# Preparing the hidden layers' weights in the first batch of a fused attention, Fourier and feed-forward kernel

## The reference

```python
q_d, k_d, v_d = means of q, k, v over groups of 4 tokens          # 144 rows
out_up    = repeat(softmax(q_d @ k_d.T / 8) @ v_d, 4)
out_local = softmax(band |i - j| < 4 of q @ k.T / 8) @ v
x  = heads side by side of (out_up + out_local)                   # 576 x 512
u  = x + real(fft over tokens, then over columns)
un = (u - mean(u)) / sqrt(var(u) + 1e-6)
y  = u + relu(un @ w_ch1) @ w_ch2                                 # 512 x 2048, 2048 x 512
gate = sigmoid(causal 5-tap convolution of y, per column)
out  = (gate * (y @ w_val)) @ w_out
```

## Time and profile before

| what | us |
|---|---|
| three timed runs | 818.84, 819.88, 823.23 |
| their median | 819.88 |
| the profiled execution, whole | 816.47 |
| its span, first to last instruction | 814.7 |
| first matmul of the hidden layers starts | 140.17 |

### The profile page before, as it was taken

The page is one execution under the profiler, slowest core; times in us unless marked ns, Lnnn a source line. Parts: engine busy times, 40 slices in busy tenths (PEclk is TensorE's granted clock), DMA queues, the critical chain, the costliest instruction groups (busy, mean ns, idle before and its releaser), DMA issues.

```text
span 814.7 us, 15570 instructions
## 1 busy us (share of the span) xinstructions
PE 728.4 (89%) x5956; PEld 542.8 (67%) x5956; DVE 436.8 (54%) x955; ACT 204.7 (25%) x409; POOL 65.3 (8%) x82
## 2 busy tenths in 40 slices
PE   1838546799999998999999998999999999999998
PEld 1624225577776776787776776777776777777776
DVE  6838769744453585644553584643643681113552
ACT  1206585222221122222221122222211122111101
POOL 3000213000110210000100210000100210000000
PEclk9999555999999999999999999999999999999999
DMA  9991031702200103602200204513100000000001
GB/s 285 285 254 46 2 130 54 170 9 71 62 1 1 59 30 105 127 12 75 48 1 1 59 30 131 104 29 79 26 2 1 0 30 30 2 1 1 1 15 45
DMA packets 42106, 49.15 MB, mean 60 GB/s; under 512 B 4784, under 2 KB 35568, under 8 KB 40944
## 3 DMA queue, kind: packets, MB, share of 16 engines
q1 hardware_dynamic: 33392, 31.69, 16.1%
q10 hardware_dynamic: 8640, 16.43, 6.2%
HBM read 43.38 MB, written 4.72 MB: 59 GB/s over the span
## 4 chain that ended last, share of the span: by engine, by line
PE 72%; DVE 11%; DMA 6%; issue 6%; ACT 3%; POOL 1%; SPq 1%; ACTq 0%; DVEq 0%; POOLq 0%
PE P L499 21%; PE Y L515 21%; PE P L622 4%; PE Y L611 4%; PE Y L622 3%; PE A L524 3%; DMA kl<-qk_win 2%; PE A L486 2%; DMA shared<-v_pool 2%; PE A L479 2%; PE A L469 2%; PE A L411 1%; PE A L572 1%; PE A L422 1%; PE A L566 1%
## 5 line engine op out<-in xcount | busy, mean ns | idle before, releaser
L499 PE MATMUL P<-unT,w 128*128 128x288 f16 x1536 | 210.0, 287 | 8.7 <-issue 4.8
L515 PE MATMUL Y<-hT,w 128*128 128x288 f16 x1536 | 214.9, 286 | 1.5 <-DVE xT L1068 1.5
L1047 DVE SCALAR_TENSOR_TENSOR hT<-P,hT 128x288 f16<-128x288 f32 x128 | 58.3, 456 | 259.1 <-ACT hT L728 259.1
L499 PEld LDWEIGHTS P<-unT,w 128*128 128x128 f16 x1536 | 148.4, 98 | 52.4 <-issue 12.2
L515 PEld LDWEIGHTS Y<-hT,w 128*128 128x128 f16 x1536 | 144.8, 98 | 45.6 <-issue 7.0
L728 ACT ACTIVATE hT<-P 128x288 f16<-128x288 f32 x128 | 52.5, 410 | 193.5 <-PE P L499 193.4
L1083 DVE SCALAR_TENSOR_TENSOR gate<-xT,cw,gate 128x288 f32<-128x288 f32 x128 | 66.4, 519 | 4.5
L699 ACT ACTIVATE prob_or_un<-prob_or_un 73x288 f32<-73x288 f32 (+1 forms) x52 | 23.3, 449 | 141.4 <-DVE prob_or_un L918 141.4
L524 PE MATMUL A<-sdft,pair_or_folded 128*128 128x289 f32 (+5 forms) x102 | 32.7, 443 | 8.7 <-DVE pair_or_folded L975 8.7
L622 PE MATMUL P<-shared,wo 128*128 128x288 f32 x128 | 32.1, 409 | 0.7 <-DVE shared L1095 0.5
L622 PE MATMUL Y<-shared,wo 128*128 128x288 f32 x128 | 32.1, 409 | 0.5 <-DVE shared L1095 0.5
(11 more groups left out here) (147 smaller groups left out, 831.4 us busy)
## 6 DMA issues: line engine op xcount, KB each, us to landing
w<-w_ch ACTq DMA_DIRECT2D x8, 1024.0 KB, 12.0
kl<-qk_win SPq DMA_DIRECT2D x40, 140.0 KB, 5.2
ql<-qk_win SPq DMA_DIRECT2D x20, 256.0 KB, 4.9
vl<-v_win SPq DMA_DIRECT2D x72, 65.0 KB
pair_or_folded<-qk_pool SPq DMA_DIRECT2D x8, 580.0 KB, 4.9
pair_or_spectrum<-qk_pool SPq DMA_DIRECT2D x8, 580.0 KB, 5.3
out<-ot ACTq DMA_DIRECT2D x32, 144.0 KB, 1.8
x<-v_pool SPq DMA_DIRECT2D x4, 576.0 KB
```

Of the source, the lines that this page charges most:

```text
L499: last = mm(P[s % 2][:, 0:HN], w1s[:, k, f * 128:(f + 1) * 128, wt], unT[:, ut, k, ha * HN:(ha + 1) * HN], start=k == 0 and wt + ut == 0, ...
L515: last = mm(Y[d][:, 0:HN], w2s[:, f, d * 128:(d + 1) * 128, wt], hT[s % 3][:, ht, :], start=f == 0 and wt + ht == 0, stop=f == KF - 1 and ...
L1047: nc.vector.scalar_tensor_tensor(out=hT[s % 3][:, 1, :], in0=P[s % 2][:, 0:HN], scalar=0.0, in1=hT[s % 3][:, 0, :], op0=ALU.max, op1=ALU.s ...
```

## The change

- *Scales.* In place of the greatest magnitude, the sum of squares of the whole matrix sets the power of two. ScalarE squares each chunk into a scratch tile and accumulates the row sums (`weight_square`), in its slots 4 to 15 and around the spectrum copies. PE adds them over partitions with a matmul of ones (`weight_sum`), and DVE makes the scale in five operations. The exponents 5 and 13 become 10 and 14.
- *w1.* It is loaded two chunk places further on in a wider tile, so that a chunk's two halves, now side by side, go two places ahead and need no temporary and no copy. ScalarE makes the high halves. DVE makes the low halves of chunks 0, 2, 4, 6 in one operation each; GpSimd those of 1, 3, 5, 7 in two operations (scale, subtract), one before the folds and one after each of them. w_val is loaded into the last two places once w1 is split.
- *w2.* GpSimd alone splits it, after the last 1/sqrt, in four operations a chunk. The down matmuls now wait by chunk: hidden tile 0 for one chunk, tile 2 for two, tile 4 for four, tile 8 for all eight.
- *Values.* In the first batch GpSimd sums the value tiles in two additions each. Before that it does one very early tensor_tensor on a constant. The loop steps keep DVE's reduce.
- *Keys.* The third window of the first batch has its own buffers for queries and keys, in the tile that held the second value tile; GpSimd clears the key buffer once the values are summed. On SP's queue the value windows 3 and 4 come before the key windows 4 and 5. The identity has its own semaphore and is loaded earlier.
- *Weight loads.* w1 in ScalarE's slots 1 to 4; w2 in 7, 8, 13 and 14, and the transform tables in 13.

```diff
-HID_BITS, W2_BITS = 5, 13
+HID_BITS, W2_BITS = 10, 14
...
-POOLING_FIRST = {1: [("qk", 1)], 2: [("v", 0)], 3: [("v", 1), ("qk", 2)], 5: [("qk", 3)]}
-WEIGHT_LOADS = [2, 3, 4, 5, 6, 7, 9, 10, 8]
+POOLING_FIRST = {1: [("qk", 1)], 3: [("qk", 2)], 5: [("qk", 3)]}
+WEIGHT_LOADS = {1: [0], 2: [1], 3: [2], 4: [3], 7: [4], 8: [5], 13: [8, 6], 14: [7]}
+SQUARES = {4: 0, 5: 1, 6: 2, 7: 3, 8: 4, 9: 5, 10: 6, 11: 7, 12: 8, 13: 9, 14: 10, 15: 11}
+W1_HIGH = {12: [0, 1], 13: [2], 14: [3], 15: [4], 16: [5]}
+W1_LOW = {13: 0, 14: 2, 15: 4}
+W2_NEEDED = {0: 1, 2: 2, 4: 4, 8: 8}
 SEQ_AT, FEAT_AT = 24, 29
-W1_AT = 11
+W1_AT = 12
...
+def keys(b, t):
+    if opening(b) and t == 2:
+        return ql_first, kl_first, ld_qk_first, 1
+    i = (0, 1, 0, 0, 1)[t] if opening(b) else t % 2
+    if opening(b):
+        return ql[i][:], kl[i][:], ld_qk[i], (1, 1, 1, 2, 2)[t]
+    return ql[i][:], kl[i][:], ld_qk[i], b * (3 - i) + t // 2 + i
...
 def wchunk(c, part=None):
-    w, ws = ((w1, w1s), (w2, w2s))[c // WCH]
     if part is None:
-        return w[:].rearrange("p k f -> p (k f)")[:, c % WCH * WCW:(c % WCH + 1) * WCW]
-    return ws.rearrange("p k f t -> p (k f) t")[:, c % WCH * WCW:(c % WCH + 1) * WCW, part]
+        return w1_wv[:, c + 2, :] if c < WCH else w2c[:, c - WCH, :]
+    return (w1h if c < WCH else w2h)[:, c % WCH, (1 - part) * WCW:(2 - part) * WCW]
...
+        if opening(b):
             window(b, 2, "v")
-        window(b, 2, "qk")
-        window(b, 3, "qk")
-        if not later(b):
             window(b, 3, "v")
+            window(b, 3, "qk")
             window(b, 4, "qk")
             window(b, 4, "v")
         else:
+            window(b, 3, "qk")
             window(b, 2, "v")
...
-        if what == "v" and opening(b):
-            done = UD + 1 if t == 4 else 0
+        if opening(b):
+            done = (UD + 1 if t == 4 else 0) if what == "v" else (0, 0, 0, UD + 1, UD + 2)[t]
...
         if what == "qk":
-            sp.dma_start(ql[i][:], qk_win[b, t, :, :, 0:128]).then_inc(ld_qk[i], 16)
+            q_tile, k_tile, landed, _ = keys(b, t)
+            if opening(b) and t == 2:
+                sp.wait_ge(zeroed, 7)
+                sp.sem_inc(passed, 1)
+            sp.dma_start(q_tile, qk_win[b, t, :, :, 0:128]).then_inc(landed, 16)
             for j in range(2):
-                sp.dma_start(kl[i][D * j:D * j + D, :, j, :], qk_win[b, t, D * j:D * j + D, :, 128:128 + 2 * WK]).then_inc(ld_qk[i], 16)
+                sp.dma_start(k_tile[D * j:D * j + D, :, j, :], qk_win[b, t, D * j:D * j + D, :, 128:128 + 2 * WK]).then_inc(landed, 16)
         else:
             tile, landed, _ = values(b, t)
...
+            if s in W2_NEEDED:
+                pe.wait_ge(w2_split, W2_NEEDED[s])
             if s == 0:
-                pe.wait_ge(w_split, 2 * WCH)
                 pe.wait_ge(step_over, b + 1)
...
+    def weight_sum(i):
+        pe.wait_ge(w_squares, WCH * (i + 1))
+        mm((A[0], P[0])[i][:, 0:WCH], one.to_broadcast([128, 128]), wsum[:, i, :], start=True, stop=True).then_inc(w_all, 1)
...
+                if s == W1_AT:
+                    weight_sum(0)
...
                 mix_feat(b, j)
+                if j == 0:
+                    weight_sum(1)
...
+            w, dram = ((wv, w_val), (wo[:], w_out))[c - 2 * KD - 1]
+            if c == 2 * KD + 1:
+                for done in w1_split:
+                    act.wait_ge(done, WCH // 2)
+            act.dma_start(w, dram.rearrange("(k p) f -> p k f", p=128)).then_inc(ld_wvo, 16)
...
     def weight_high(c):
-        i = c // WCH
-        if c % WCH == 0:
-            act.wait_ge(w_scale, i + 1)
-        nc.scalar.activation(wtmp[:, c % 2, :], wchunk(c), ACT.Copy, scale=wscale[:, i:i + 1]).then_inc(w_high, 1)
-    def weight_in_place(c):
-        act.wait_ge(w_low, c + 1)
-        nc.scalar.copy(wchunk(c, 0), wtmp[:, c % 2, :]).then_inc(w_split, 1)
-    def weights(c):
+        if c == 0:
+            act.wait_ge(w_scale, 1)
         if c >= 2:
-            weight_in_place(c - 2)
-        if c < 2 * WCH:
-            if c >= 2:
-                act.wait_ge(w_split, c - 1)
-            weight_high(c)
+            act.wait_ge(w1_split[c % 2], c // 2)
+        nc.scalar.activation(wchunk(c, 0), wchunk(c), ACT.Copy, scale=wscale[:, 0:1]).then_inc(w_high, 1)
+    def weight_square(c):
+        if c % 2 == 0:
+            act.wait_ge(ld_w[c // 2], 16)
+        if c > 0:
+            act.wait_ge(w_squares, c)
+        nc.scalar.activation(gate[:].rearrange("p d c -> p (d c)")[:, 0:WCW], wchunk(c), ACT.Square,
+                             accum_out=wsum[:, c // WCH, c % WCH:c % WCH + 1]).then_inc(w_squares, 1)
     def gate_e(b, ha):
         act.wait_ge(tap_done, 8 * TAPS * b + 4 * TAPS * (ha + 1))
...
             if m is None:
-                if s in WEIGHT_LOADS:
-                    load_weights(WEIGHT_LOADS.index(s))
+                for c in WEIGHT_LOADS.get(s, []):
+                    load_weights(c)
...
-            if m is None and W1_AT <= s < W1_AT + WCH:
-                weights(s - W1_AT)
+            if m is None:
+                for c in W1_HIGH.get(s, []):
+                    weight_high(c)
+                if s in SQUARES:
+                    weight_square(SQUARES[s])
...
                 gate_e(m, 0)
         if m is None:
-            for c in range(S0 + NU + LAG_AV - W1_AT, WCH):
-                weights(c)
-            load_weights(2 * KD + 1)
-            load_weights(2 * KD + 2)
-            for c in range(WCH, WCH + 4):
-                weights(c)
+            for c in range(WCH + 4, WCH + 6):
+                weight_square(c)
             for g in range(5):
                 spectrum(b, g)
+            for c in range(WCH + 6, 2 * WCH):
+                weight_square(c)
+            for c in range(6, WCH):
+                weight_high(c)
+            load_weights(2 * KD + 2)
             for j in range(3):
-                weights(WCH + 4 + j)
                 odd_part(b, j)
+            load_weights(2 * KD + 1)
             for i in range(6):
                 u_columns(b, i, m)
-                if i == 1:
-                    weights(WCH + 7)
                 un_columns(b, i)
-            for c in range(WCH + 8, 2 * WCH + 2):
-                weights(c)
...
     def weight_scale(i):
         dve.wait_ge(w_all, i + 1)
-        t = wtop[:, 1, i:i + 1]
+        t = wtop[:, i:i + 1]
         sc = wscale[:, i:i + 1]
+        nc.vector.tensor_reduce(t, (A[0], P[0])[i][:, 0:WCH], axis=AX.X, op=ALU.add).then_inc(w_chain, 1)
+        dve.wait_ge(w_chain, 5 * i + 1)
         nc.vector.tensor_scalar(t, t, 2.0 ** -100, None, ALU.max).then_inc(w_chain, 1)
-        dve.wait_ge(w_chain, 3 * i + 1)
-        nc.vector.tensor_scalar(t.bitcast(u32), t.bitcast(u32), 0x7F800000, None, ALU.bitwise_and).then_inc(w_chain, 1)
-        dve.wait_ge(w_chain, 3 * i + 2)
+        dve.wait_ge(w_chain, 5 * i + 2)
+        nc.vector.tensor_scalar(t.bitcast(u32), t.bitcast(u32), 1, 0x7F800000, ALU.logical_shift_right,
+                                ALU.bitwise_and).then_inc(w_chain, 1)
+        dve.wait_ge(w_chain, 5 * i + 3)
         nc.vector.reciprocal(sc, t).then_inc(w_chain, 1)
-        if i == 1:
-            nc.vector.tensor_scalar(unscale[:], wtop[:, 1, 0:1], t, 2.0 ** -(HID_BITS + W2_BITS), ALU.mult, ALU.mult)
-        dve.wait_ge(w_chain, 3 * i + 3)
-        nc.vector.tensor_scalar(sc, sc, 2.0 ** (HID_BITS, W2_BITS)[i], None, ALU.mult).then_inc(w_scale, 1)
+        dve.wait_ge(w_chain, 5 * i + 4)
+        nc.vector.tensor_scalar(sc, sc, 2.0 ** ((HID_BITS, W2_BITS)[i] - 64), None, ALU.mult).then_inc(w_scale, 1)
+        if i == 0:
+            dve.sem_inc(w_chain, 1)
+        else:
+            dve.wait_ge(w_scale, 2)
...
-        i = c // WCH
-        nc.vector.scalar_tensor_tensor(out=wchunk(c, 1), in0=wchunk(c), scalar=wscale[:, i:i + 1],
-                                       in1=wtmp[:, c % 2, :], op0=ALU.mult, op1=ALU.subtract).then_inc(w_low, 1)
+        nc.vector.scalar_tensor_tensor(out=wchunk(c, 1), in0=wchunk(c), scalar=wscale[:, 0:1], in1=wchunk(c, 0),
+                                       op0=ALU.mult, op1=ALU.subtract).then_inc(w1_split[0], 1)
     def hidden_low(b, s):
...
             if m is None:
-                if W1_AT - 6 <= s < W1_AT - 2:
-                    weight_max(2 * (s - W1_AT + 6))
-                    weight_max(2 * (s - W1_AT + 6) + 1)
-                if s == W1_AT - 2:
-                    weight_top(0)
-                if s == W1_AT - 1:
+                if s == W1_AT:
                     weight_scale(0)
...
-                if W1_AT <= s < W1_AT + WCH:
-                    if s > W1_AT:
-                        weight_low(s - W1_AT - 1)
-                    weight_max(s - W1_AT + WCH)
-                if s == W1_AT + WCH:
-                    weight_low(WCH - 1)
-                    weight_top(1)
+                if s in W1_LOW:
+                    weight_low(W1_LOW[s])
         if m is None:
```

(63 more changed lines are left out.)

81 lines of the change are left out of this document (47 added, 34 removed).

## The result

The changed kernel takes 812.75 us (median of 5 runs, 809.6 to 813.45) against 819.88 us (5 runs) on the same chip: ratio 0.9894, 95% interval 0.9866 to 0.9922. It is 7 us faster; the forecast had 20. The profiled execution took 811.06 us, its span is 809.2 us.

The account below looks back on a forecast made before the run. Bound: the first batch's waits before the loop, PE being busy 650.6 of the 674.5 us after. Sum 816.5 - 19.9 + 1 - 1 = 796.6 for the profiled run, 800 us as a median; range 782 to 816.

Parts of the forecast that it names:

- the way to the third output: Start to the first batch's third local output copied: at 70.5 us instead of 77.06, gain 6.6.
- M to T0: From the feature transform's start (M) to the first loop matmul (T0): 25.6 us instead of 24.9.
- the loop head: Loop entry: VectorE pools the next batch without its last w2 pass, 1.4 us, partly taken back by the value load: -1.
- Values on GpSimd: First batch: pooled values at 23.3 us, 2.7 us lost, with 7.3 us taken for GpSimd's first tensor_tensor.
- Scales from squares: First batch: squares of 1.1 us on ScalarE, PE steps of 2.95 us, seven steps and a transpose ending at 46.5.
- Third key buffer, w2 later: First batch: third window's keys by 46, 11.7 us wait goes; fourth's at 55.8, some 3 us late; gain 6.6.
- The queue rival: First batch: the key wait only moves, SyncE's queue being full; 6 us more late, 806 to 809 us; chance 0.11.
- w1 split: Third output to last fold: 18 us instead of 20.7 (14 to 21), folds end at 88.5; gain 2.7.
- w2 off ScalarE and DVE: Last fold to feature transform: 6.2 us instead of 17.5, gain 11.3, transform at 94.7.
- w2 on GpSimd: Around loop entry: 6.2 us a chunk, eight done at T0+45.1, just before slot 10 needs them; 1 us charged.
- 8c − 4.5 − 46.6: PE's wait at loop slot 10 for c us a w2 chunk: nothing up to 6.4, the whole gain from 8.9.
- the mild rival: w2 chunks of 7 to 8.5 us on GpSimd add 5 to 17 us at slot 10: 805 to 817; chance 0.13.

Follow-up runs that it names:

- the repeated run: The changed kernel once more, unchanged: median 813.7 us, ratio 0.991 to the kernel before.
- the best version: Changed kernel with w1's low halves on VectorE, first w1 loads a slot later, w2 scaled on ScalarE, two key buffers, first w2 chunk held back: 793.5 us.

## Why the prediction was wrong

It had the direction and the largest term, and overstated the gain almost three times: 20 us for 7. Three of its terms missed by 3.7 to 3.8 us each (the way to the third output, M to T0, the loop head), and the one for w2 by 1.5. By its own steps:

- *Values on GpSimd.* Pooled at 21.0 instead of 23.3: the first tensor_tensor took 0.20 us, not 7.3. Of no use, as raw pair 3 landed at 26.5 us, 19.2 us after its issue, beside w1's four loads. I had w1's earlier loads only hold up SyncE; that they hold up the raw pairs was missing. The first local transpose ended at 49.5, not 46.5. With the loads a slot later it ended at 41.9, but then the third window's keys landed at 48.7, not by 46.
- *Scales from squares.* 1.04 us and 0.19 us for reading the sum, as expected, and steps of about 2.9 us.
- *Third key buffer, w2 later.* Failed in the attribution, which I gave to both together. The later loads alone take the wait from 11.7 to 2.3 us. The fourth window's wait was forecast right (3 us, measured 2.8), with its keys at 58.6 and not 55.8. The queue rival, given 0.11, holds for what comes next: with the raw pair early, the wait moves to the third window again (6.8 us). In the profiled runs M comes 3 to 5 us earlier with two buffers and the old order; the medians (0.987 against 0.989) don't tell them apart. There PE reached the higher clock level (at 62.95 us a product of 1.12 us that took 2.08 in the changed kernel); whether that is the cause wasn't tried.
- Together the third output came 3.8 us later than forecast (74.26 against 70.5), 3.0 of them there by the first local transpose.
- *w1 split.* 19.1 us against 18, right for the wrong price: scaling 2.85 us against the 1.2 taken and a bound of 2.1. A low half took 5.1 us alone and 6.8 and 5.6 between the folds, where 3.4 to 6 were allowed. That the sum came out is luck in part.
- *w2 off ScalarE and DVE.* M 5.1 us behind the folds, forecast 6.2: right. But M to T0 took 29.3, not 25.6. Of the 4.4 us over the kernel before, chunk 7 is 1.5 (29.3 to 27.8 in two versions; 0.7 were forecast for it), GpSimd's scaling beside VectorE's last normalisation 2.1, and 0.8 are not traced. I had priced GpSimd's operations and asked who waits for their results; I hadn't asked what they do to the VectorE pass that merely runs at the same time, though the rule stood in my next paragraph.
- *w2 on GpSimd.* 7.23 us a chunk by the scaling's price; my own formula, 8c − 4.5 − 46.6, gives 6.7 us of wait, measured were 2.4 and 3.8, because GpSimd starts 6.1 us ahead of T0 instead of 4.5 and PE itself asks 3 us later. This is the mild rival's price, given 0.13, at a smaller wait than its 5 to 17 us. (The forecast's own operations add up to 6.1 us a chunk, not 6.2.)
- *Loop head: −1.* The sign was wrong. From T0 the up-projections of slot 5 come 25.0 us later against 22.1 before (23.7 in the repeated run): +2.8 where I had −1. I had VectorE gain 1.4 us by the w2 pass that it no longer makes, and the value load behind it take back a part. It took back more than all: the tile is issued 0.9 us ahead of T0 in both kernels, but VectorE's reduction of it starts at T0 + 4.4 before and at T0 + 6.4 after (T0 + 5.2 in the repeated run), and the third up-projection waits behind that. VectorE's and PE's timelines before:

```profile
144.53 3.62 DVE L900 TENSOR_REDUCE vd<-x 72x512 f32<-72x2048 f32 x1 [0.59 <-DMA x<-v_pool]
```

```profile
148.58 1.65 PE L499 MATMUL P<-unT,w 128*128 128x288 f16 x12 [3.21 <-DVE hT L1047]
```

  VectorE's timeline after:

```profile
134.13 3.65 DVE L950 TENSOR_REDUCE vd<-x 72x512 f32<-72x2048 f32 x1 [3.88 <-DMA x<-v_pool]
```

  The third group itself took 3.06 us instead of 1.65. With w2's wait (2.4) the entry costs 5.4 us where I had 0; all of T0 to the end costs 7.0 (11.4 in the repeated run), and the 1.6 us behind slot 12 are not traced.

Of the 14.4 us missing in the span, 3.8 lie ahead of the third output, 3.7 between M and T0, 7.0 behind T0, and the two terms between cancel (1.1 each).

Open: why the next batch's value tiles take longer to land after an earlier T0, the versions without a w2 wait included (slot 5 at T0 + 24.9 in the best version, where PE waits for a unit behind the second tile). The first tile takes at most 5.2 us in the kernel before and 7.3 in the changed one, the second 8.6 in the kernel before and 9.9 and 10.7 in the last combined version and in the one with later loads only. Whether their neighbours on the DMA engines or their issue time decide wasn't tried.

## What to carry to other kernels

When a load is late, first ask what else is on the DMA engines between its issue and its landing, and move that; a buffer helps only where the issue itself waits. Where one engine's work is handed to another, price the operation in its exact form and list what runs beside it, not only who waits for its result. A gain ahead of a loop is worth only what the loop's next-latest supplier leaves of it: here each 1 us at T0 needed w2 to be 1 us faster too. And when one edit of many is cheap to make alone, run it alone first: three numbers in a load table gave all that the median of the whole change shows.

## What was not expected of the hardware

On GpSimd a scaling of 128x1024 fp32 by one number per partition takes 2.85 us and the same product of two tensors 1.89 us; a copy to fp16 takes 1.04 us. A gap of 7.1 to 7.5 us stood ahead of GpSimd's first two-input operation behind the first reduction over partitions in three versions that have one, though 32 to 42 us and two memsets lay between. And after the same wait PE's third up-projection ran at different levels: with chunk 7 on VectorE 3.06 us (granted clock 0.50 over 134.5 to 137.6 us), in the last version 1.64 us (1.00 over 121.4 to 123.1). The 24 matmuls ahead of the wait had taken 5.26 us there and 4.50 us here. PE's timelines of the two:

```profile
134.51 3.06 PE L539 MATMUL P<-unT,w_wv 128*128 128x288 f16 x12 [3.16 <-DVE hT L1095]
```

```profile
121.44 1.64 PE L534 MATMUL P<-unT,w_wv 128*128 128x288 f16 x12 [3.16 <-DVE hT L1099]
```
